# Routing in groups of four tiles with one region per expert, and another order of attention's work

## What is computed

```python
# attention: 4 batches x 8 heads, 768 steps, heads of 48
for t in range(S):
    y[:, :, t] = einsum('bhd,bhde->bhe', q[:, :, t], state)
    v_old = einsum('bhde,bhd->bhe', state, kt)              # kt: normed key
    state = state + beta * einsum('bhd,bhe->bhde', kt, vt - v_old)
# experts: 8 of 384 -> 1024 -> 384, each token goes to the best one
logits = normed(x) @ normed(expert_emb).T / tau
expert_idx = argmax(logits, axis=1); gate = softmax(logits)[expert_idx]
for e in range(8):
    out[expert_idx == e] = gate * (relu(x[expert_idx == e] @ w1[e]) @ w2[e])
# dense: 384 -> 2048 -> 384
h = x @ w_in;  g = where(h > 0, h, exp(min(h, 0)) - 1);  out = g @ w_out
```

## Time and profile before

| | |
|---|---|
| median of 3 runs | 1016.96 us (1016.02 to 1019.41) |
| the profiled execution: its time | 1017.75 us |
| its span, first to last instruction | 1016.0 us |
| mean granted TensorE clock | 0.954 |
| PE busy | 893.6 us (88%) |
| DVE, ACT, POOL busy | 564.9, 562.9, 238.2 us |

### The profile page before, as it was taken

How to read it: one execution, slowest core, us unless ns; L and a number is a source line. 1 busy time by engine, 2 the same in 40 slices (tenths; PEclk the granted TensorE clock), 3 DMA queues, 4 the chain that set the end, 5 groups by cost and what they waited for, 6 DMA issues and landing times. The chain is left out here.

```text
span 1016.0 us, 27418 instructions
## 1 busy us (share of the span) xinstructions
PE 893.6 (88%) x11523; PEld 609.7 (60%) x11523; DVE 564.9 (56%) x998; ACT 562.9 (55%) x1045; POOL 238.2 (23%) x291
## 2 busy tenths in 40 slices
PE   3798998999969305999999999999999999999995
PEld 3787887888865104666766676555555555555553
DVE  7676776786644635666556632544444444444442
ACT  3676776777735334666666643545454454544542
POOL 5466676656541171000000000001001010000101
PEclk9799999999997756999999999999999999999998
DMA  7143333333100177544544400000000000000000
GB/s 286 49 129 111 120 124 113 107 104 96 38 2 2 63 257 272 154 142 152 156 145 147 136 1 2 1 1 32 1 1 33 1 31 0 8 23 0 32 1 31
DMA packets 38109, 78.81 MB, mean 78 GB/s; under 512 B 3816, under 2 KB 26480, under 8 KB 38000
## 3 DMA queue, kind: packets, MB, share of 16 engines
q1 hardware_dynamic: 34928, 67.77, 21.2%
q0 software_dynamic: 3072, 9.45, 2.5%
HBM read 67.76 MB, written 9.45 MB: 76 GB/s over the span
## 5 line engine op out<-in xcount | busy, mean ns | idle before, releaser
L1408 PE MATMUL bankH<-rows_or_y,wd 128*128 128x512 f16 (+1 forms) x864 | 201.8, 379 | 1.7 <-PEq L1047 1.7
L1420 PE MATMUL bankO<-wd,gd_hi 128*128 128x384 f16 x768 | 187.4, 326 | 0.6
L1408 PEld LDWEIGHTS bankH<-rows_or_y,wd 128*128 128x128 f16 x864 | 84.5, 98 | 93.6 <-issue 1.8
L1420 PE MATMUL bankO<-wd,gd_lo 128*128 128x384 f16 x384 | 125.2, 326 | 0.0
L655 DVE CAST_PREDICATED merge<-pair_mask,bankA 128x512 f16<-128x512 uint16 x120 | 85.4, 711 | 65.1 <-PE bankA L379 64.9
L1420 PEld LDWEIGHTS bankO<-wd,gd_hi 128*128 128x128 f16 x768 | 74.6, 98 | 62.1 <-DVE gd_lo L1482 2.8
L1505 POOL DMA_INDIRECT out<-o_rows,dest x24 | 25.1, 1047 | 347.2 <-ACT o_rows L1459 235.3
L1475 DVE SCALAR_TENSOR_TENSOR gd<-hd_exp,hd 128x512 f32<-128x512 f32 x96 | 66.5, 692 | 66.8 <-ACT hd_exp L1445 66.8
L1482 DVE SCALAR_TENSOR_TENSOR gd_lo<-gd,gd_hi 128x512 f16<-128x512 f32 x96 | 66.5, 693 | 64.4 <-ACT gd_hi L1453 64.4
L1453 ACT ACTIVATE gd_hi<-gd 128x512 f16<-128x512 f32 x96 | 60.5, 630 | 69.1 <-DVE gd L1475 68.2
L1443 ACT ACTIVATE hd<-bankH 128x512 f32<-128x512 f32 x96 | 57.3, 596 | 71.7 <-PE bankH L1408 71.6
(11 more groups left out here) (199 smaller groups left out, 1639.1 us busy)
## 6 DMA issues: line engine op xcount, KB each, us to landing
kq_t<-in_kq_rows SPq DMA_DIRECT2D x24, 512.0 KB, 4.4
stage<-in_moe_w SPq DMA_DIRECT2D x24, 512.0 KB
stage<-in_moe_w SPq DMA_DIRECT2D x32, 384.0 KB
k_tok<-in_k_pad SPq DMA_DIRECT2D x24, 384.0 KB, 3.1
rows_or_y<-x_sorted SPq DMA_DIRECT2D x12, 385.0 KB, 8.1
k_norm<-in_k_tok SPq DMA_DIRECT2D x24, 192.0 KB, 4.3
v_in<-in_v_tok SPq DMA_DIRECT2D x24, 192.0 KB, 2.4
stage<-in_moe_w_in SPq DMA_DIRECT2D x8, 384.0 KB
```

Source lines behind the costliest of these rows:

```text
L1408: last = nc.tensor.matmul(h_bank[f % 4][:, :], wd1[:, a, c, P * f:P * f + P], y_t[:, b, c, bass.ds(blk * NB, NB)], start=c == a == b == 0, ...
L1420: last = nc.tensor.matmul(o_bank[s][:, 0:DM], (g_lo if a else g_hi)[:, f % 4, P * s:P * s + P], wd2[:, b, f, :], start=f == a == b == 0, s ...
```

## The change

In attention the same steps stand in another order on PE, ACT, DVE and POOL, `kq_t` has six slots, and three things are added: ACT sums the squares of each finished row tile (`square_rows`), SP writes zeros to 24 stretches of 256 rows in DRAM (`zero_rows`), and SP loads embeddings and `tau`. `route` goes; `experts` holds the routing now. It takes the tiles in six groups of four: for each group logits, one-hot, gate, and places (a running base per expert is carried on), after which POOL scatters the four tiles to `regions`, where expert e owns rows from `CAP * e`. When the last group is placed, DVE writes one word an expert (`shares_i`: start and further rows packed); SP writes 128 rows of zeros behind each expert's rows, waits for these and for all scatters, and loads for each expert a fourth tile into `more_rows` (memory of expert 1's `we2`) and three tiles into `xrows`. `lay_out` transposes them in order of experts to the column where each begins: in a loop the tiles beyond three (at least one), then the three fixed ones, which the next expert overwrites where they reach too far. Behind every turn of that loop POOL loads a further tile of the expert. The token numbers go to DRAM by 24 indirect DMAs of their own, and SP loads `perm` from there. With these inputs the experts hold 351 to 434 rows, so that each loop of `lay_out` runs once.

```diff
-KQ = 5
-SQUARE = 8
-XW = DM + 1
+KQ = 6
+SQUARE = 9
...
+            def zero_rows(n):
+                e, j = n // (ZEROED // 2), 2 * (n % (ZEROED // 2))
+                sp.dma_start(regions[CAP * e + P * j:CAP * e + P * j + 2 * P, :].rearrange("(t p) d -> p t d", p=P),
+                             pers["zeros"][:].unsqueeze(1).to_broadcast([P, 2, DM])).then_inc(s_zeroed, 16)
...
+            def square_rows(it):
+                act.wait_ge(s_o, it.n + 1)
+                need(act, s_sq, it.n)
+                nc.scalar.activation(row_sq[:], xrows[:, it.n], ACT.Square,
+                                     accum_out=pers["ss"][:, it.n:it.n + 1]).then_inc(s_sq, 1)
...
+            sp.wait_ge(s_shares, 1)
+            for e in range(E_N):
+                word = sp.value_load(shares_i[0:1, e:e + 1], min_val=STATIC * P + 1 - BASE, max_val=(NTOK << 12) + NTOK)
+                row = ((word & 4095) + (BASE + CAP * e)).with_bounds(min_val=CAP * e, max_val=CAP * e + NTOK)
+                sp.dma_start(regions[bass.ds(row, P), :], zeros[:]).then_inc(s_zeroed, 16)
+            sp.wait_ge(s_zeroed, 16 * E_N)
             sp.wait_ge(s_sc, 16 * NT)
-            for t in range(0, NT, LOADED):
-                sp.dma_start(xrows[:, t:t + LOADED, :], x_sorted[P * t:P * (t + LOADED), :]
-                             .rearrange("(t p) w -> p t w", p=P)).then_inc(s_row[t // LOADED], 16)
-            for e in range(1, E_N):
+            for e in range(E_N):
+                sp.dma_start(more_rows[:, e, :],
+                             regions[CAP * e + STATIC * P:CAP * e + (STATIC + 1) * P, :]).then_inc(s_row[e], 16)
+                sp.dma_start(xrows[:, STATIC * e:STATIC * e + STATIC, :],
+                             regions[CAP * e:CAP * e + STATIC * P, :].rearrange("(t p) w -> p t w", p=P)).then_inc(s_row[e], 16)
+            for j in range(NPC):
+                if j == 3:
+                    sp.wait_ge(s_loaded, 1)
+                stage_piece(1, j, True)
+            sp.wait_ge(s_ids, 16 * NT)
+            sp.dma_start(perm[:], ids.rearrange("(t p) w -> p (t w)", p=P), allow_slow_non_contiguous=True).then_inc(s_perm, 16)
+            for e in range(2, E_N):
                 for j in range(NPC):
                     stage_piece(e, j, True)
...
+            for e, (_, _, _, first, count) in enumerate(at):
+                with pool.Fori(0, count) as i:
+                    pool.wait_ge(s_mtp, first + i + 1)
+                    row = (i * P + (CAP * e + (STATIC + 1) * P)).with_bounds(min_val=CAP * e, max_val=CAP * e + NTOK)
+                    nc.gpsimd.dma_start(more_rows[:, e, :], regions[bass.ds(row, P), :]).then_inc(s_further, 16)
+                    pool.wait_ge(s_further, (first + i) * 16 + 16)
+                    nc.gpsimd.tensor_tensor(prime[:, 4:5], ident[:, 0:1], ident[:, 0:1], ALU.mult).then_inc(s_more[e % (E_N // 2)], 1)
+                    pool.wait_ge(s_more[e % (E_N // 2)], (at[e - E_N // 2][4] if e >= E_N // 2 else 0) + i + 2)
+            nc.gpsimd.memset(prime[:, 4:5], 0.0).then_inc(s_loaded, 1)
+            pool.wait_ge(s_final, 1)
+            for t in range(NT):
+                nc.gpsimd.indirect_dma_start(
+                    out=ids, out_offset=bass.IndirectOffsetOnAxis(ap=final[:, t:t + 1], axis=0),
+                    in_=tok_id[:, t:t + 1], in_offset=None).then_inc(s_ids, 16)
...
+            for g in range(GROUPS):
+                logits_back(g)
+                if g + 1 < GROUPS:
+                    logits(g + 1)
+                if g + 2 < GROUPS:
+                    turn_tiles(g + 2)
+                ranks(g)
...
+            for g in range(GROUPS):
+                exponentials(g)
+                gate_rows(g)
+                if g + 1 < GROUPS:
+                    keep_logits(g + 1)
+                if g + 2 < GROUPS:
+                    for t in range(GT * (g + 2), GT * (g + 3)):
+                        keep_turned(t)
+                high(0, g)
...
+            def more_tile(e, k, i, col):
+                act.wait_ge(s_mtp, k + 1)
+                need(act, s_tl, STATIC * e)
+                nc.scalar.copy(x_t[:, 0, :, bass.ds(col, P)],
+                               more_bank[:, 0:DM].rearrange("p (c n) -> p c n", c=DC)).then_inc(s_mth, 1)
...
```

More of the change, by code:

```diff
@@ L504, in body @@
                 if n2.exists():
-                    freed(pe, s_x[3], n2.after(-1))
-                    merged_x(n2, 0)
+                    freed(pe, s_yv[3], n2.after(-1))
+                    merged_y(n2, 0)
                 if n3.exists():
@@ L774, with experts @@
 COLS = NTOK + GROUP + TAIL
+STATIC = 3
+MORE = -(-(NTOK - STATIC * P) // P)
+CAP = NTOK + P
+ZEROED = 6
+BASE = GROUP + 1 - TAIL
+XCOLS = NTOK + (STATIC + 1) * P
 SC = 1024.0
-def route(nc, pers, expert_emb, tau):
-    xrows, ident = pers["xrows"], pers["ident"]
-    tiles, pos_i, gate = pers["tiles"], pers["place"], pers["gate"]
+def experts(nc, pers, regions, ids, w1, w2, w_in, w_out):
+    xrows, ident, en_t, emb, tau_in, ss = (pers[n] for n in ("xrows", "ident", "en_t", "emb", "tau", "ss"))
+    zeros, perm, wd1, wd2 = (pers[n] for n in ("zeros", "perm", "wd1", "wd2"))
+    y_t = pers["rows_or_y"][:, :].bitcast(F16).rearrange("p (a c n) -> p a c n", a=2, c=DC)
     GT = 4
@@ L1040, in experts @@
-def experts(nc, pers, x_sorted, w1, w2, w_in, w_out):
-    xrows, ident, tiles, place, gate = (pers[n] for n in ("xrows", "ident", "tiles", "place", "gate"))
-    perm, wd1, wd2 = (pers[n] for n in ("perm", "wd1", "wd2"))
-    y_t = pers["rows_or_y"][:, :].bitcast(F16).rearrange("p (a c n) -> p a c n", a=2, c=DC)
-    ctx = ExitStack()
-    with ctx:
-        def sb(name, shape, dt=F32):
-            return ctx.enter_context(nc.sbuf_tensor(name, shape, dt))
-        def sem(name):
-            return ctx.enter_context(nc.semaphore(name))
-        x_t = sb("xs_t", [P, 2, DC, COLS], F16)
+        ones16 = sb("ones16", [P, P], F16)
@@ new lines, in experts @@
+        tot = sb("tot", [P, E_N])
+        pos_f = sb("pos_f", [P, NT])
+        place = sb("place", [P, NT], I32)
+        pos_c = sb("pos_c", [P, 2, NT])
+        final = sb("final", [P, NT], I32)
+        ends = sb("ends", [P, 6, E_N])
+        shares_i = sb("shares_i", [P, E_N], I32)
+        x_t = sb("xs_t", [P, 2, DC, XCOLS], F16)
+        early = x_t[:, 1, 0, 0:NTOK].bitcast(F32)
+        emb_sq = early[0:E_N, 0:384]
+        before = early[:, 384:512]
+        l_t = early[:, 512:640]
+        work = early[:, 640:832].rearrange("p (s t e) -> p s t e", s=6, t=GT)
@@ new lines, in logits @@
+            def logits(g):
+                if g == 0:
+                    pe.wait_ge(s_xta, 2)
+                    pe.wait_ge(s_xtd, 2)
+                    pe.wait_ge(s_en, 1)
+                else:
+                    pe.wait_ge(s_xta, 2 + GT * g)
+                    pe.wait_ge(s_lt, g)
+                for c in range(DC):
+                    for j in range(GT):
+                        last = nc.tensor.matmul(lt_bank[LW * j:LW * j + LW, 0:P], en_t[:, c, :],
+                                                turned[:, g % 2, c, P * j:P * j + P], start=c == 0, stop=c == DC - 1,
+                                                skip_group_check=True)
+                last.then_inc(s_lp, 1)
@@ new lines, in _ @@
+            turn_tiles(0)
+            pe.wait_ge(s_emb, 4)
+            for c in range(DC):
+                last = nc.tensor.transpose(l_bank[:, 8 * c:8 * c + 8], emb[:, P * c:P * c + P], ident[0:E_N, 0:E_N])
+            last.then_inc(s_et, 1)
+            logits(0)
+            turn_tiles(1)
+            for g in range(GROUPS):
[5 more added lines that the diff above has]
+                ranks(g)
@@ L1185, in _ @@
                 last.then_inc(s_tp, 1)
-            pe.wait_ge(s_tl, NT)
+            def more_tile(e, k, i, col):
+                pe.wait_ge(s_mtl, k + 1)
+                pe.wait_ge(s_row[e], 32)
+                pe.wait_ge(s_more[e % (E_N // 2)], (at[e - E_N // 2][4] if e >= E_N // 2 else 0) + i + 1)
+                for c in range(DC):
+                    last = nc.tensor.transpose(more_bank[:, P * c:P * c + P], more_rows[:, e, P * c:P * c + P], ident[:])
+                last.then_inc(s_mtp, 1)
```

719 lines of the change are left out of this document (376 added, 343 removed).

## The result

The changed kernel takes 1059.74 us (median of 4 runs, 1056.46 to 1061.48) where the kernel before takes 1017.99 (4 runs on the same chip): ratio 1.0412, with a 95% interval of 1.0386 to 1.0438. Forecast were 1012.5 us and a range up to 1027. The profiled execution's span is 1054.8 us, 38.8 more than before.

The account below looks back on a forecast made before the run. PE was taken as the limit in attention, experts and dense, but not in the 96.4 us between attention and experts. Terms -8 - 17.5 + 7.3 + 13 = -5.2 against 1017.75 us gave 1012.5 us, range 998 to 1027.

Parts of the forecast that it names:

- attention's order: Attention: the new order saves 0.35 us an item over 24 items, term -8 us, bounds nothing to 14 us.
- the way to the rows: From attention's last output to the first transpose of sorted rows: 62.3 us instead of 79.8, term -17.5 (-24 to -8).
- the layout: Transposing sorted rows: 2.9 us an expert, 24 us for eight against 16.8, term +7.3 us.
- the queue behind POOL: Experts 0 and 1: further loads and token-number scatters delay `perm` and weight pieces, 11.5 and 1.5 us lost, term +13.
- POOL's turn: Layout: POOL's load of one further tile with its waits takes 3.8 us, between 3.0 and 5.3, eight times.
- the 0.59 us: Attention: PE's idle time for DVE's copy of the level before, expected to stay.
- the 0.26 us: Attention: a PE wait, 0.26 us an item, expected to go since `merged_x` and `merged_y` of level 0 stand earlier.
- The bound of nothing: Attention: the lower bound of the gain, nothing saved per item, against 0.6 us an item at the upper.
- The first group's places: Routing: the first group's chain of embeddings, norms, logits, transposes and ranks takes 13.9 us.
- A group: Routing: each of five more groups takes 5.7 us, including some 1.1 of DVE waiting, 28.6 us together.
- SP's eight words: Before the row loads: SP reads eight words and issues a write each, 1.15 us apiece, 9.2 us in all.
- POOL falls behind: Rival, chance 0.20: POOL's further-tile load takes 5.3 us among the row loads, so the kernel is slower at 1024.5 us.

Follow-up runs that it names:

- e4: The kernel before with only attention's new order on all four engines, without squares of rows, zero writes or new routing: 1015.8 us, ratio 1.0.
- e12: The changed kernel without the squares of attention's output rows on ACT, their sums set to one: 1059.8 us, ratio 1.0417.
- e8: The changed kernel with DVE subtracting the low half of the previous group's weight piece instead of the current one's: 1056.9 us, ratio 1.0401.
- e9: The changed kernel minus further loads, SP's eight words and zeros, PE's last further-tile wait; `perm`, token numbers, weight piece later; ACT's further-tile copies earlier: 1047.0 us.
- e2: The changed kernel without POOL's eight loads of a further tile and PE's waits for them: 1038.2 us, ratio 1.0221.
- e1: The changed kernel with SP loading `perm` after all weight pieces of experts 2 to 7: 1047.6 us, ratio 1.034.
- e7: The changed kernel without POOL's further loads, `perm` last on SP, token-number scatters held until all experts' weight pieces are split: 1060.8 us, ratio 1.0448.
- e13: e10 with POOL's 24 token-number scatters and the load of `perm` moved to the start of the dense stage: 1023.7 us, ratio 1.0057.
- e14: e13 made complete for any row count: further loads behind a branch, SP's eight words and zero writes back but later: 1023.5 us, ratio 1.0056.
- e10: e9 with the token-number scatters spread, four in each of experts 0 to 5, instead of in one row: 1020.9 us, ratio 1.0051.

## Why the prediction was wrong

Four terms of the sum failed: attention's order, -8 for 0; the way to the rows, -17.5 for -8.6; the layout, +7.3 for +17.4; and, the largest miss, the queue behind POOL, +13 for +28.2, in which POOL's turn was priced at 3.8 us, at most 5.3, and took 5.8.

- **What bounds the kernel.** Right: the whole loss lies between attention and expert 2, where PE waits.
- **Attention, -8.** Wrong, 0. That the 0.59 us stays was right. That "the 0.26 us goes" and gives 0.35 an item is the step that failed: undisturbed items come 10.73 us apart instead of 10.77, and e4 measures 0 +- 2 us for all. The trace of the changed kernel shows the 0.26 in front of another step, where PE waits for DVE to empty bankA0. The prediction's reason, that `merged_x` and `merged_y` of level 0 stand earlier, is about what stood ahead of the wait; the waiting step, `off_diagonal` of level 1, needs the copies of DVE and ACT. The bound of nothing was in the text, with the wrong reason beside it: in e12 the squares cost nothing that can be told.
- **Up to the first sorted transpose, -17.5.** Measured -8.6. The first group's places took 18.1 us from the last output to POOL's first scatter, not 15.6. A group is 6.9 us, not 5.7 (5 x 1.2 = 6.0 us): DVE stands behind ACT's weight piece, and PE behind ACT's copies (e8), for which the sum had 1.1 us of waiting. SP's eight words were priced well (1.1 to 1.2 us each), and e9 shows that they hold the loads back by 7.4 us. The PE clock of 0.61 to 0.64 lies between the two that the text gave; its own part was not measured.
- **Layout, +7.3.** Measured 32.9 us, 16.1 above. Missed: PE's further tile of expert e waits for POOL's load of expert e - 4. That isn't the largest part: with these loads gone 32.1 of the 35.7 us to the first relu are left (e2). The rest is the relay from ACT to DVE and back, some 3.3 us an expert in e2, which I had at 2.9, and the 3.5 us that PE idles ahead of the first expert's matmul, 1.8 of them with register sums for a wait. e9 takes 6.8 us of both away.
- **The queue behind POOL, +13.** The mechanism was there as the prediction told it: ACT idle at expert 2's first piece, expert 1's fourth piece late. The size was not, and a second mechanism was missing. POOL's turn is 5.8 us, beyond the upper bound of 5.3. Its row of 2.7 us was taken with DMA engines nearly empty; here POOL waits 2.1 us for a load in the quiet part and up to 5.9 in the crowd, and is idle for another 1.5 to 2.7 us ahead of each, in part put down to issue. The term came to 28.2 us (11.2 and 17.0). With `perm` last 15.8 of them are left (e1), without POOL's further loads 8.9 (7.8 and 1.1, e2), and with the scatters of token numbers away as well 0.9 (e7). These last 8 us are the missing mechanism: weight pieces land late beside the scatters.
- **The rule of the Trainium skill** ("DMA: Bandwidth & Descriptors", Anatomy of one DMA) gave 2.45 us for such a load. The trace agrees in the quiet part (an issue of 0.55 us and 2.1 to 2.2 of idle time behind it, 2.7 together) and not beside the row loads (5.7 and 6.5 together).
- **The rival "POOL falls behind"**, given 0.20 and 1024.5 us, names what happened. It stopped at its own bound of 5.3; with 5.8 it gives 8 x 2.0 = 16 us more than the forecast, 1028.5. Of the 44.0 us between the forecast difference (-5.2) and the spans' (+38.8), 7.8 are attention, 8.9 the way to the rows, 10.1 the layout, 15.2 the queue and 2 the rest: every term missed to the same side, and the range was made as if they were independent.

## What to carry to other kernels

For each wait that a new order is to remove, ask which result the waiting step needs, and not only what stands ahead of it: here the 0.26 us went along to the step's new place. Price a turn of load, landing and release by a row from the same crowd of transfers, and if there is none let the upper bound be open: eight turns multiply the error. For each item of a serial relay list which engine holds the token, and give each a row in the sum; ACT in the groups and POOL in the layout had none, and both lengthened it. Work that is never needed can still cost 20 us by what stands behind it, so look first at where each queue's idle pieces, here `perm`, are wanted last.

## What the runs showed of the hardware

- While POOL scatters 4-byte elements (24 times 128, 12 KB in 31 us), a weight piece of 384 KB lands after 8.8 us (e2) in place of 3.4 (e7, without them) to 3.7. The DMA share is 0.45 then, for 66 GB/s; with no scatters it is 0.38 for 117 GB/s.
- The same row of scatters can hold up PE's short matmuls: 108 in 30.5 us (e7), also in e8 and e9, with the idle time put down to issue, on ACT too. It starts 2.4 us behind the first scatter in e7 and e9, some 14 in e8, and ends 3 to 5 us behind the start of the last. In the changed kernel and in e1 the same scatters met a tail without it (2.26 us for 72 matmuls). What decides is open, and so is the resource. PE's matmuls of 512 columns keep their pace beside the same row (32.45 of 32.5 us busy, e13), but ACT stands still for 6.4 us around its end, and PE's matmuls come 1.9 us late behind that, in e13 and e14 alike.
- The 24 scatters of rows of 1,536 bytes, while PE ran its small transposes and logits, show none of it in the changed kernel: PE's idle time put down to issue sums to 1.0 us between 326 and 362.
- Register sums for waits are not free on PE: 16 register operations for one wait take some 1.8 us (L1175), within 3.5 us of idle time ahead of the first expert's matmul; that wait less is part of e9's 6.8 us.
- POOL's drain at the end of the dense stage takes 2.01 us, and 4.07 in e13 and e14, where the scatters of token numbers and the load of `perm` stand in that stage.
- PE idles 0.44 us ahead of the second turn of an unedited loop of 144 matmuls, or 1.6 us where only code around it had changed (e10, e13, e14). The Trainium skill ("Runtime: NRT & Kernel Launch", Instruction fetch mechanics) says that each engine fetches its program in blocks of 16 KiB through a DMA queue of its own, and that a taken branch to a block not at hand waits for the fetch. That would fit this and the starved stretches; no run here shows it. In the trace of e7 the instruction queues have 3 packets between 596 and 650, while PE stops some 20 times, so that a fetch for each stop is not what it shows.
